# Row sums of tiles 1 to 3 one pair of heads later, first expert step one head later, clock fillers behind the product with V

## What is computed

```python
# attention: batch 2, 8 heads, 576 rows, head size 64
scores = scale * q @ k.T
kth = np.partition(scores, -32, axis=-1)[..., -32:-31]
attn = softmax(np.where(scores >= kth, scores, -1e9))
x = (attn @ v)                        # to 1152 tokens x 512
# experts: P = exp(x @ w_gate - max), 8 times divided by row sums, then by column sums
for e in range(8):
    out += P[:, e:e+1] * (np.maximum(x @ w1[e], 0) @ w2[e])    # 512 -> 1024 -> 512
# last layer, 512 -> 2048 -> 512
h = x @ w_in
y = (h * np.tanh(np.log1p(np.exp(h)))) @ w_out
```

## Time and profile before

| | us |
|---|---|
| median of 3 runs | 1416.5 |
| lowest, highest | 1414.52, 1420.11 |
| profiled execution | 1411.53 |
| its span, first to last instruction | 1409.7 |
| busy: PE, DVE, ACT, POOL | 1355.8, 750.3, 616.4, 448.8 |

### The profile page before, as it was taken

The page is one execution under the profiler, slowest core; times in us unless marked ns, Lnnn a source line. Parts: engine busy times, 40 slices in busy tenths (PEclk is TensorE's granted clock), DMA queues, the critical chain, the costliest instruction groups (busy, mean ns, idle before and its releaser), DMA issues.

```text
span 1409.7 us, 20196 instructions
## 1 busy us (share of the span) xinstructions
PE 1355.8 (96%) x7204; PEld 1169.1 (83%) x7204; DVE 750.3 (53%) x1379; ACT 616.4 (44%) x1146; POOL 448.8 (32%) x255
## 2 busy tenths in 40 slices
PE   7989999999999999679999999999999998999998
PEld 6777788788888889578998899988999887898776
DVE  4978887678879770162122313131322223888775
ACT  3444455656666564232222222222222223788675
POOL 1332445444545557353222322223222231000000
PEclk8999999999999999889999999999999999999999
DMA  8020112322222223232212121312222111222230
GB/s 131 19 76 1 39 59 70 95 93 79 87 82 82 76 97 114 71 103 94 68 52 97 45 97 46 110 61 80 82 74 82 60 60 46 74 76 76 75 123 35
DMA packets 139696, 105.22 MB, mean 75 GB/s; under 512 B 34288, under 2 KB 116208, under 8 KB 139632
## 3 DMA queue, kind: packets, MB, share of 16 engines
q1 hardware_dynamic: 139632, 104.37, 24.2%
HBM read 96.49 MB, written 7.86 MB: 74 GB/s over the span
## 4 chain that ended last, share of the span: by engine, by line
PE 79%; ACT 9%; DVE 9%; issue 2%; DMA 0%; POOL 0%; SPq 0%; DVEq 0%
PE ps L468 29%; PE ps L483 29%; PE ps L413 6%; PE ps L392 6%; PE ps L492 4%; PE ps L403 3%; ACT m_d L844 2%; ACT m_r L847 2%; ACT m_a L842 2%; DVE m_r L1057 1%; DVE m_a L1054 1%; ACT m_r L849 1%; DVE m_a L1060 1%; ACT h_hi L856 1%; DVE work L909 1%
## 5 line engine op out<-in xcount | busy, mean ns | idle before, releaser
L1147 POOL TENSOR_TENSOR w_lo<-w_raw,w_hi 128x1024 fp32r<-128x1024 f32 x130 | 314.1, 2417 | 418.4 <-ACT w_hi L684 418.4
L993 DVE SCALAR_TENSOR_TENSOR h_lo<-ps,h_hi 128x384 fp32r<-128x384 f32 x128 | 71.1, 557 | 378.1 <-ACT h_hi L824 378.1
L468 PE MATMUL ps<-x_hi,w_hi 128*128 128x384 f32 x768 | 267.6, 348 | 2.2 <-DVE acc L979 2.2
L468 PE MATMUL ps<-x_hi,w_lo 128*128 128x384 f32 x768 | 261.9, 341 | 0.0
L468 PE MATMUL ps<-x_lo,w_hi 128*128 128x384 f32 x768 | 261.1, 340 | 0.0
L824 ACT ACTIVATE h_hi<-ps 128x384 fp32r<-128x384 f32 x128 | 62.9, 492 | 410.9 <-PE ps L468 410.9
L684 ACT ACTIVATE w_hi<-w_raw 128x1024 fp32r<-128x1024 f32 x160 | 168.2, 1052 | 0.1
L468 PEld LDWEIGHTS ps<-x_hi,w_hi 128*128 128x128 f32 x768 | 146.1, 190 | 23.4 <-issue 10.2
L907 DVE MAX8 top<-work 128x8 f32<-128x576 f32 x216 | 152.3, 746 | 0.0
L483 PE MATMUL ps<-w_hi,h_hi 128*128 128x512 f32 x384 | 152.1, 396 | 0.0
L483 PE MATMUL ps<-w_lo,h_hi 128*128 128x512 f32 x384 | 151.4, 394 | 0.0
(11 more groups left out here) (109 smaller groups left out, 2241.1 us busy)
## 6 DMA issues: line engine op xcount, KB each, us to landing
w_raw<-in_moe_w SPq DMA_DIRECT2D x256, 256.0 KB, 3.0
w_raw<-in_moe_w_in SPq DMA_DIRECT2D x32, 256.0 KB, 2.8
w_raw<-in_moe_w_out SPq DMA_DIRECT2D x32, 256.0 KB, 3.1
spill<-y_out SPq DMA_DIRECT2D x7, 768.0 KB, 3.8
y_in<-spill SPq DMA_DIRECT2D x7, 768.0 KB, 4.3
qraw<-in_q SPq DMA_DIRECT2D x18, 128.0 KB, 3.0
vones<-in_v SPq DMA_DIRECT2D x8, 256.0 KB, 5.5
out<-acc SPq DMA_DIRECT2D x8, 256.0 KB, 2.8
```

Source lines behind the costliest of these rows:

```text
L468: last = nc.tensor.matmul(ps[:, bank, 0:BT], wt[:, s, 0, c * P:(c + 1) * P], xt[:, c, blk * BT:(blk + 1) * BT], start=(n == 0), stop=(n == ...
L993: v_.scalar_tensor_tensor(out=h_lo[:, s, :], in0=ps[:, HB_BANK + j, 0:BT], scalar=0.0, in1=h_hi[:, s, :], op0=ALU.max, op1=ALU.subtract).t ...
L1147: g_.tensor_tensor(w_lo[:, s, :, :].rearrange("p a n -> p (a n)"), w_raw[:, s, :, :].rearrange("p a n -> p (a n)"), w_hi[:, s, :, :].rearr ...
```

## The change

Six edits, made together:

- VectorE, tiles 1 to 3: both row sums of the tile before are taken in the second pair of heads instead of the first, again between the pair's last MAX8 and its mask.
- TensorE and ScalarE: the transposition of x and its copies stand in slot 5 instead of slot 4 (`X_AT`).
- The first expert step stands in slot 5 of tile 3 instead of slot 4 (`LAG` = 5). All later steps move one slot back, so that 47 steps and not 48 are done when attention ends; the logits start one step earlier, and the Sinkhorn iterations keep their steps.
- The clock fillers stand behind the product with V. In slots 0 to 3 of tile 0, which have no such product, there are none any more; slot 4 of tile 3 has them now.
- GpSimd, tiles 1 and 2: mask of head 1, the two multiplications, mask of head 3, subtraction, masks of heads 5 and 7.
- The helper `tile` of GpSimd is written out.

```diff
--- before.py
+++ after.py
@@ -180,7 +180,8 @@
             return T * H + h
 
 
-        LAG = 4
+        LAG = 5
+        X_AT = 5
         FILLERS = 8
 
         def chunk_at(T, h):
@@ -188,7 +189,7 @@
             e, f = (T - MIX, h + NF - LAG) if h < LAG else (T - MIX + 1, h - LAG)
             return (None, None) if isinstance(T, int) and e < 0 else (e, f)
 
-        AFTER = (NT - MIX) * NF + H
+        AFTER = (NT - MIX) * NF + H + 4 - LAG
         LOGITS = AFTER + 2
         SINKHORN = E * NF - ITERS
         LOGIT_CHUNKS = -(-NT * DC * 2 // (3 * DC + 3 * BLK))
@@ -435,7 +436,7 @@
                     expert, f = chunk_at(T, h)
                     if keys and 2 <= h <= KC + 1:
                         pe.wait_ge(k_copied, KC + h - 1)
-                    if early and before is not None and h == 4:
+                    if early and before is not None and h == X_AT:
                         x_transposed(T - 1)
                         pe.wait_ge(x_copied, T)
                     if late_parts is not None:
@@ -443,8 +444,6 @@
                     scores(T, h, parts)
                     if expert is not None:
                         up_a(expert, f)
-                    else:
-                        keep_clock()
                     if following and h == H - 1:
                         queries_transposed(T + 1)
                     if isinstance(T, int) and T == 0 and h == 4:
@@ -452,6 +451,8 @@
                         pe.wait_ge(v_in[0], 16 * KC)
                     if late_parts is not None:
                         attend(late, (h - 4) % H, late_parts)
+                        if expert is None:
+                            keep_clock()
                     if not early and h == H - 1:
                         if following:
                             pe.wait_ge(q_copied, T + 2)
@@ -756,7 +757,7 @@
                 for h in range(H):
                     late, late_on = (T - 1, before) if h < 4 else (T, True)
                     expert, f = chunk_at(T, h)
-                    if early and before and h == 4:
+                    if early and before and h == X_AT:
                         x_copy(T - 1, two_before)
                     if late_on:
                         probs_copied(late, (h - 4) % H)
@@ -919,7 +920,7 @@
 
             def tile_body(T, before=True):
                 for pair in range(NPAIR):
-                    if before and T < MIX and pair == 0:
+                    if before and T < MIX and pair == 1:
                         pair_masked(T, pair, lambda: (row_sums(T - 1, 0), row_sums(T - 1, 1)))
                     else:
                         pair_masked(T, pair)
@@ -1136,12 +1137,6 @@
                 g_.tensor_tensor(x_lo[:, :, bass.ds(T * P, P)], x_f[:, :, :], x_hi[:, :, bass.ds(T * P, P)],
                                  ALU.subtract).then_inc(x_split, 1)
 
-            def tile(T, reused=True):
-
-                normalised(T, 0, reused)
-                normalised(T, 1, reused)
-                x_low(T)
-
             def split_lo(step, s):
                 pool.wait_ge(w_hi_done, step + 1)
                 g_.tensor_tensor(w_lo[:, s, :, :].rearrange("p a n -> p (a n)"),
@@ -1177,13 +1172,20 @@
 
 
             for T in range(POOL_TILES):
+                mask(T, 1)
                 if T > 0:
-                    tile(T - 1, reused=T > 1)
-                for h in range(1, H, 2):
-                    mask(T, h)
+                    normalised(T - 1, 0, reused=T > 1)
+                    normalised(T - 1, 1, reused=T > 1)
+                mask(T, 3)
+                if T > 0:
+                    x_low(T - 1)
+                mask(T, 5)
+                mask(T, 7)
             for f in range(AHEAD):
                 split_lo(A0 + f, f % RING)
-            tile(POOL_TILES - 1)
+            normalised(POOL_TILES - 1, 0)
+            normalised(POOL_TILES - 1, 1)
+            x_low(POOL_TILES - 1)
             for h in range(LAG, H):
                 chunk_a(*chunk_at(MIX - 1, h))
             with pool.Fori(MIX, NT) as T:
```

## The result

| | before | changed |
|---|---|---|
| median of 12 runs each, us | 1414.38 | 1421.66 |
| lowest, highest | 1407.81, 1420.11 | 1417.97, 1428.66 |
| ratio, 95% interval | | 1.0056 (1.0038 to 1.0074) |
| span of the profiled execution | 1409.7 | 1419.3 |

The change costs about 7.3 us (1421.66 − 1414.38), 0.5%, which is the edge of what the prediction calls measurable; the interval (0.4 to 0.7%) leaves out zero. The forecast was 1422.3. The number is right; its terms are less so.

What follows compares the result with a forecast made beforehand. TensorE (PE) was taken to bound the kernel, by how late it comes to its work. Terms 1.4 + 2.0 + 2.7 + 1.9 − 1.2 + 0 − 1.0 = +5.8 us on 1416.5 gave 1422.3; range 1412 to 1429.

Steps and rivals of the forecast that it cites:

- Waits for `xn`: TensorE before the transposition of x: near 2, 4 and 4.6 us in tiles 1 to 3, 10 to 11 total instead of 5.3.
- Tile 3: Wait before the transposition 4.6 us against 1.9, VectorE masking both heads: +2.7; fillers in slot 4 counted separately, +1.9.
- The ring: TensorE's scores let VectorE begin a pair, VectorE's results let TensorE go on four slots later; nearly level, 5.10 against 5.19 us.
- Tile 0: Empty slots 0 to 3: slot 4 starts 2.9 us earlier but runs at half clock for 3.2 more; taken as 0.
- the slower rival: Half clock lasts through slot 5 of tile 0, +2.4, and costs fully in tiles 2 and 3, +1.0: 1425.7 us, chance 0.16.
- The clock: Tiles 2 and 3 together: the clock falls partly before TensorE comes back, so less work lies in it, −1.0 us.
- tile 2: Transposition starts at 133.3, TensorE is done with slots 1 to 4 at 129.4 and waits 3.9 us against 1.9: +2.0.
- Tile 1: Wait before the transposition grows by 0.65 us, and the copy's 0.7, hidden before, is now paid: +1.4.
- The later first step: Slot 4 of tile 3 has fillers as new work, the expert step being done later at full price: +1.9 us.
- The fillers: Behind the product they leave ScalarE time to copy: 0.11 us per slot, about eleven slots in tiles 0 to 2, −1.2.
- GpSimd's two halves: GpSimd's multiplications, having both halves at once, add 0.2 us to the 1.63 from second row sum to transposition.
- The late part: From 184 us on, steps moved by one: same TensorE work, Sinkhorn waits may fall differently; 0, ends −2.4 and +2.4 us.

Runs made afterwards that it cites:

- f1: The kernel before with the fillers alone moved behind the product with V, slots 0 to 3 of tile 0 keeping theirs: 1403.64 us, ratio 0.9936.
- f2: f1 without fillers in slots 0 to 3 of tile 0: 1402.75 us, ratio 0.9942 to the kernel before.
- h1: The changed kernel timed again, side by side with h2 on one chip: 1423.89 us, ratio 1.0079 to the kernel before.
- h2: The changed kernel with fillers put back in slots 0 to 3 of tile 0, on the same chip as h1: 1421.88 us, ratio 1.0074 to before.
- f4: The kernel before with LAG = 5 alone, the first expert step in slot 5 of tile 3: 1414.86 us, ratio 1.0016.
- g1: One more execution of the unaltered changed kernel, for a second look at its timeline: 1430.75 us.
- g4: The changed kernel with row sums, transposition and GpSimd's order as before (f2 and LAG = 5): 1406.92 us, ratio 0.9969 to the kernel before.
- g2: The changed kernel with 7, 15 and 24 more fillers behind slot 4 of tiles 1, 2 and 3: 1418.13 us, ratio 1.0056 to the kernel before.
- f3: The changed kernel with fillers in slots 0 to 3 of tile 0 again: 1424.98 us, ratio 1.0099 to the kernel before.

## Why the prediction came out right

- **Waits for `xn`: right.** Predicted 10 to 11 us in total, about 2, 4 and 4.6; measured 11.4, as 1.83, 3.70 and 5.86. The first two are good to 0.3. Tile 3's is 1.3 longer: DVE also waits 1.34 us for the exponentials of head 1 before it can mask (at 180.62), which the term left out. The ring was read rightly: DVE's wait in the middle of tile 2 is 6.31, at least 4 as foretold.
- **Tile 0: wrong, 0 predicted, +2.6 measured.** DVE's second MAX8 (17.84) and PE's slot 4 (27.69) came where they were expected, 17.8 and 27.7. But the half clock, which was to cost 3.2, cost 4.46 in slot 4 (9.56 instead of 5.10) and 1.14 in slot 5 (6.24). That is the point at which the slower rival was to decide, with its +2.4, and here the rival's term is the one that came. The Trainium skill, "TensorE: Matmul & The Clock Gate", "What's actually happening", says that the throttled state is the default and activity releases it; here 0.50 stood until nearly 40 us, where before it had gone by 24, so the trace agrees with it. Yet the runs with and without these fillers (f1 and f2, h1 and h2) show no difference in the median that can be told. The +2.6 is one pair of profiles: tile 1 starts between 51.09 and 54.66 us in the six others with fillers in slots 0 to 3 and between 52.67 and 54.75 in the five others without, because in those six the clock fell again in slot 4.
- **The clock: wrong sign.** I took −1.0, because part of the half clock would fall into the wait. But the half clock itself became longer, 13.7 us and not 6.8. In tile 2 it cost 4.46 in slot 5, 1.03 in slot 6 and 0.3 in the transposition, 5.8 in all against 3.2 before: +2.6. So tile 2 gave +4.4 (1.8 of it the wait), not +2.0. In tile 3 the same adds about 1.3: 16.8 − 9.6 = +7.2 there, against +4.6 (2.7 and 1.9).
- **Tile 1: +2.6** against +1.4, a mis-sized term. The wait grew by 0.4; the rest is half clock, slot 5 lasting from 87.77 to 98.49.
- **The later first step: right.** +1.9 predicted, +2.5 in f4 alone (0.6 to 4.0 by its interval).
- **The fillers: −1.2 predicted, nothing measured, and the reason missed.** I counted 0.11 us per slot for an earlier copy. The transposed probabilities do take 0.60 instead of 0.71, but the product with V takes 1.47 instead of 1.37, and a slot lasts 5.09 instead of 5.10 (43.49 to 48.58). I did not see that behind the product they cover the way of the last product to `xn`, which in the kernel before is worth 9 us (f1). Here the row sums wait for DVE's own second pair, and it is worth nothing. The early profile agrees: DVE's waits on `rsum` went, and PE gained nothing.
- **GpSimd's two halves: right.** They took 1.70 us together, against 0.61 for one alone, and DVE's mask beside them 1.12 instead of 0.80. x came 1.92 after the second row sum was taken (136.52 to 138.44); 1.83 was predicted. The Trainium skill, "SBUF — State Buffer", "Who interferes with whom", has the first to issue hold up the other; the mask, which starts 0.11 us after GpSimd's first half and takes 0.32 longer, agrees.
- **The late part: predicted 0, and not told apart from 0.** The profile's −6 us belongs to one execution. Reduction to `x_lo` took 598.35, 604.0 and 604.2 us in three profiles of the changed kernel, and 600.85 to 605.5 in the six others with the later step; 599.6 and one step, 4.5, is 604.1.

So in the profile the attention part lost 16.8 us and not 5.8, and the first expert matmul came at 198.97 where the prediction had about 188. The 11.0 between them are: tile 0 2.6, tile 1 1.2, tile 2 2.4, tile 3 2.6, and the two gains that I had counted and that did not come, 1.2 and 1.0. By that the forecast should have been 1416.5 + 16.8 = 1433, and two later profiles of the changed kernel, at 1430.75 (g1) and 1428.13 (h1), against 1411.53 of the one of before, do lie 17 to 19 us apart. The medians lie 7.3 and 11.3 (h1) apart. Part of this is that the one profile of before is one of the shorter executions of its kernel (3 us under the session's 1414.38), and g1 and h1 are long ones of theirs (4 to 9 us above 1421.66 and 1423.89); the first profile of the change, at 1421.07, was near its median only because its late part was 6 us short. Which landmarks move in the executions between, which have no profile, stays open. The forecast's size was right partly by luck: its waits and its later step hold, its clock does not, nor its two gains.

## What to carry to other kernels

If an engine must be kept busy with work that nobody reads, put it behind the last instruction on which others wait, not ahead of it: there it covers their latency, and here that was worth 9 us of 1412 (f1). Before a consumer is moved later to rid one engine of a wait, compare when the engine behind it arrives; removing 3.5 us of idle time per tile on VectorE, which was not the bound, made TensorE's waits 0.4 to 3.9 us longer, and its time at half clock on top. Profile the same kernel again before a stretch that is 6 us shorter is put down to a change.

## What the hardware showed that was not expected

**The clock's fall isn't settled by the gaps alone.** Gaps of 0.69 and 1.18 us, and of 1.17 alone, kept 1.00 in f1; f2, with the same ones, fell once and g4 twice; g2, with 0.35 to 0.69 and 1.18, fell in all three tiles; and the changed kernel had 17.1 us at half clock in tile 1 in g1 and 10.2 in its first profile. What decides it stays open. A fall cost 3.2 us in one place and 5.8 in another, so it is the price that one should carry as a range.

**Tiny instructions of VectorE are stretched beside GpSimd.** In the Sinkhorn iterations of the changed kernel (DVE, then POOL):

```profile
615.50 2.08 DVE L963 TENSOR_TENSOR gate<-gate,rows 128x72 f32<-128x72 f32 x1
...
620.36 0.23 DVE L963 TENSOR_TENSOR gate<-gate,rows 128x72 f32<-128x72 f32 x1
...
622.76 1.82 DVE L969 TENSOR_SCALAR cols<-cols 128x8 f32<-128x8 f32 x1
```

```profile
615.15 2.34 POOL L1142 TENSOR_TENSOR w_lo<-w_raw,w_hi 128x1024 fp32r<-128x1024 f32 x1
...
622.17 2.40 POOL L1142 TENSOR_TENSOR w_lo<-w_raw,w_hi 128x1024 fp32r<-128x1024 f32 x1
```

The same instruction takes 0.23 us, or 2.08 when it starts inside GpSimd's subtraction, and ends with it (617.6 and 617.5; 624.6 and 624.6). PE's waits for `gate`, 2.4 us each, number two to four from profile to profile (4.7 us here, 7.1 before, 9.5 in f3 and f4), and in g1 and h1, which are this kernel again, there are three. That their number is set by where these small instructions fall against GpSimd's is read from rows only; no run here took the subtractions away.
